# Loading and splitting the first layer's weights in another order at the start of a fused attention and MLP kernel

## What is computed

```
x = attention(q, k, v, mem_k, mem_v)   # 4 batches x 8 heads x 768 rows, head_dim 64; chunks of 32 rows,
                                       # each against 8 memory + 16 left + 32 own + 8 right keys, softmax
x = x as 3072 tokens x 512
h = x @ w_in                           # 512 x 2048
g = h * cos(h)
y = g @ w_out                          # 2048 x 512
m = max(y @ w1, y @ w2, y @ w3)        # 512 x 768 each
out = m @ w2_out                       # 768 x 512
```

## Time and profile before

| What | us |
|---|---|
| median of three runs | 960.74 |
| lowest and highest run | 957.79, 961.76 |
| the profiled execution, its own time | 957.79 |
| its span | 956.0 |
| PE busy in it | 937.4 (98%) |
| DVE busy | 678.0 (71%) |
| ACT busy | 512.6 (54%) |

### The profile page before, as it was taken

One profiled execution on the slowest core, in us unless ns is written; L12 is line 12 of the kernel. 1 busy time (PEld: TensorE's weight loads), 2 busy tenths in 40 slices (PEclk: granted clock), 3 DMA queues, 4 the chain that ended last, 5 costly groups with the idle time before them and its releaser, 6 DMA issues.

```text
span 956.0 us, 21412 instructions
## 1 busy us (share of the span) xinstructions
PE 937.4 (98%) x9100; PEld 918.7 (96%) x9100; DVE 678.0 (71%) x938; ACT 512.6 (54%) x689; POOL 183.2 (19%) x207
## 2 busy tenths in 40 slices
PE   6999999999999999999999999999999999999998
PEld 5889999999999999999999999999999999999997
DVE  5767666667666789989989889767446357677761
ACT  3879696978878894334343345433224224444541
POOL 0011211111111212001000003922000002683520
PEclk8999999999999999999999999999999999999999
DMA  8953446454653443444354343331120201335432
GB/s 302 367 190 130 154 163 212 149 189 160 203 179 124 137 168 123 154 132 156 119 196 150 113 138 97 116 122 65 60 97 34 99 34 56 129 115 171 171 111 88
DMA packets 55422, 135.60 MB, mean 142 GB/s; under 512 B 5152, under 2 KB 14368, under 8 KB 55328
## 3 DMA queue, kind: packets, MB, share of 16 engines
q1 hardware_dynamic: 44960, 98.58, 30.6%
q0 software_dynamic: 10368, 35.66, 10.3%
HBM read 87.03 MB, written 47.19 MB: 140 GB/s over the span
## 4 chain that ended last, share of the span: by engine, by line
PE 78%; ACT 8%; DVE 5%; DMA 5%; issue 2%; POOL 0%; SPq 0%; DVEq 0%; ACTq 0%
PE ps L604 25%; PE ps L606 24%; PE ps L605 24%; DMA g_dram<-work 3%; ACT work L871 2%; PE ps L645 1%; ACT work L876 1%; DVE units L1185 1%; ACT work L868 1%; PE ps L618 1%; PE ps L656 1%; ACT work L878 1%; DVE work L1148 1%; DMA early_qk<-qk_in 1%; PE ps L631 1%
## 5 line engine op out<-in xcount | busy, mean ns | idle before, releaser
L604 PE MATMUL ps<-units 128*128 128x384 f32 (+1 forms) x1940 | 607.0, 313 | 5.8 <-DVE units L1137 1.4
L606 PE MATMUL ps<-units 128*128 128x384 f32 (+1 forms) x1940 | 601.3, 310 | 0.0
L605 PE MATMUL ps<-units 128*128 128x384 f32 (+1 forms) x1940 | 601.1, 310 | 0.0
L604 PEld LDWEIGHTS ps<-units 128*128 128x128 f32 x1940 | 368.0, 190 | 10.6 <-DVE units L1089 1.7
L605 PEld LDWEIGHTS ps<-units 128*128 128x128 f32 x1940 | 368.2, 190 | 0.0
L606 PEld LDWEIGHTS ps<-units 128*128 128x128 f32 x1940 | 368.0, 190 | 0.0
L896 ACT CAST units<-work 128x1024 fp32r<-128x1024 f32 x96 | 85.8, 939 | 118.9 <-DVE work L1171 105.7
L1040 ACT COPY work<-ps 128x384 f32<-128x384 f32 (+1 forms) x144 | 63.5, 454 | 146.9 <-PE ps L606 146.7
L1185 DVE TENSOR_TENSOR units<-work,units 128x1024 fp32r<-128x1024 f32 x96 | 102.1, 1105 | 10.7 <-ACT units L896 10.7
L501 POOL DMA_DIRECT2D g_dram<-work x64 | 46.7, 729 | 300.9 <-DVE work L1148 295.2
L1148 DVE SCALAR_TENSOR_TENSOR work<-work 128x768 f32<-128x768 f32 x64 | 61.3, 958 | 39.1 <-ACT work L878 39.1
(11 more groups left out here) (91 smaller groups left out, 764.8 us busy)
## 6 DMA issues: line engine op xcount, KB each, us to landing
g_dram<-work POOLq DMA_DIRECT2D x64, 384.0 KB, 3.3
work<-g_dram SPq DMA_DIRECT2D x48, 512.0 KB, 3.7
work<-qk_in SPq DMA_DIRECT2D x18, 768.0 KB, 5.8
work<-w_in POOLq DMA_DIRECT2D x40, 256.0 KB, 4.0
h_dram<-work SPq DMA_DIRECT2D x24, 384.0 KB, 2.8
work<-h_dram SPq DMA_DIRECT2D x18, 512.0 KB, 3.8
work<-y_dram SPq DMA_DIRECT2D x8, 768.0 KB, 6.2
out<-work SPq DMA_DIRECT2D x24, 256.0 KB, 2.4
```

The source lines that it names most:

```text
L604: pe.matmul(o, wh, mh, start=start, stop=False, skip_group_check=onto)
L605: pe.matmul(o, wh, ml, start=False, stop=False, skip_group_check=onto)
L606: return pe.matmul(o, wl, mh, start=False, stop=stop, skip_group_check=onto)
```

## The change

It touches only orders; no operation is added or removed. In four places:

- **SP's queue.** The column groups 2 and 3 and the loads of pieces 3, 4 and 5 move up, the wait for the first weighted values (`pv_done`) ahead of them is gone, and the remaining groups are spread among them two by two. Each `load_qk` keeps its own wait for the scores of the piece whose buffer it takes.
- **The tables.** On ACT, column groups 6 to 15 are rounded at earlier steps, with the last at f = 4 in place of f = 9. On DVE, groups 5 to 15 move up in the same way, with the last at f = 8 in place of 10.
- **Ahead of the loop.** ACT rounds groups 2 and 3 between `x_high(0)` and `x_high(1)`. DVE does `x_low(0)` ahead of `normalise(2)` and `low_wi(1)` right behind it.
- **`normalise(n + 2)`** moves from step f = 11 to step f = 12, ahead of `x_low(n + 1)`, in blocks 0 to 6.

```
-HIGH_WI = (0, 0, 0, 0, 0, 0, 1, 1, 1, 5, 5, 5, 6, 7, 8, 9)
-LOW_WI = (0, 0, 0, 0, 0, 1, 2, 2, 3, 6, 6, 6, 7, 8, 9, 10)
+HIGH_WI = (0, 0, 0, 0, 0, 0, 0, 0, 1, 1, 2, 3, 3, 4, 4, 4)
+LOW_WI = (0, 0, 0, 0, 0, 0, 1, 1, 2, 3, 3, 4, 5, 6, 6, 8)
...
             load_v(1)
             load_v(2)
-            load_wi(0)
-            load_wi(1)
-            sp.wait_ge(pv_done, 1)
-            load_qk(NSUB)
-            load_qk(NSUB + 1)
-            for f in range(2, 6):
+            for f in range(4):
                 load_wi(f)
-            load_qk(NSUB + 2)
-            for f in range(6, 12):
-                load_wi(f)
+            for n in range(NSUB, 2 * NSUB):
+                load_qk(n)
+                load_wi(2 * n - 2)
+                load_wi(2 * n - 1)
+            load_wi(10)
+            load_wi(11)
             load_v(NSUB)
...
             x_high(0)
+            high_wi(2)
+            high_wi(3)
             x_high(1)
             x_high(2)
-            high_wi(2)
-            high_wi(3)
...
             low_wi(0)
+            x_low(0)
             normalise(2)
-            x_low(0)
+            low_wi(1)
             x_low(1)
             x_low(2)
-            low_wi(1)
             low_wi(2)
...
-                        if f == 11 and not last:
-                            normalise(n + 2)
-                        elif f == 13 and not last:
+                        if f == 13 and not last:
                             x_low(n + 2)
...
                         elif f == 12:
+                            normalise(n + 2)
                             x_low(n + 1)
```

## The result

The changed kernel is slower: 969.46 us in the median of 7 runs (963.63 to 970.4), against 960.89 of 7 runs of the kernel before (957.79 to 963.39). The ratio is 1.0075, with a 95% interval of 1.0055 to 1.0093, which is +7.2 us (5.3 to 8.9); the two medians by themselves lie 8.6 us apart. The forecast was 962.9, or +2.15, and its range ended at 967.2. A time over 965.5 had been given a chance of 0.13.

What follows compares the result with a forecast made beforehand. PE was taken to bound the kernel, with only its idle times in the first 62 us mattering. The terms +2.2 + 0.35 - 0.4 + 0 = +2.15 us on the median 960.74 gave 962.9 us, range 958.0 to 967.2.

Steps and rivals of the forecast that it cites:

- What bounds the kernel: Whole kernel: PE, busy 98% of the span; the change acts only through PE's idle time in the first 62 us.
- SP's queue, +2.2: Ahead of the loop: full DMA engines delay PE's instruction packet, new idle time near 17 us, +2.2 us, bounds 0 and 4.
- DVE ahead of the loop, +0.35: Ahead of the loop: x_low(0) first delays normalise(2) and all behind it, +0.35 us, bounds 0 and 0.6.
- The tables, -0.4: Block 0's loop: earlier rounding removes two idle times, later exponentials bring others; -0.4 us, bounds -2.06 and +0.8.
- the four priced terms: Block 0's loop: -2.06 us of idle times removed; +1.0 at turn_probs(3), +0.8 at f = 8, +0.4 at piece 4's values.
- normalise one step later, 0: Seven blocks: frees DVE for gated(4), needed only by a turn_out 2.1 us later; 0 us, bounds 0 and 7 x 0.1.
- No stop for instructions: Ahead of the loop: instructions reach PE in time, only -0.4 + 0.35 stay, 960.7 us; chance 0.25.
- All idle time of the loop won: Block 0's loop: ACT's five casts are hidden, the loop gives -2.06, no instruction stop, 959.0 us; chance 0.10.
- Stop and slow clock: Loop's start: a second idle time at 17.2 us brings PE's half clock into the first steps, 967.2 us; chance 0.15.

Runs made afterwards that it cites:

- e5: The changed kernel with WARM = 4 in place of 8, so fewer warm-up matmuls at PE's start: 968.94 us in one run.
- e3: The kernel before with SP's queue alone changed as in the change: 966.01 us, ratio 1.0031 to before.
- e4: The changed kernel with SP's wait for the first weighted values put back, behind the fourth column group: 966.75 us, ratio 1.0040 to before.
- e7: The kernel before with only DVE's order ahead of the loop as in the change: 960.26 us in one run.
- e12: The kernel before, unchanged, run for a third profile: 961.90 us.
- e2: The changed kernel with normalise(n + 2) put back to step 11: 966.56 us, ratio 1.0040 to before.
- e9: The changed kernel with normalise(n + 2) back at step 11 and SP's wait for the first weighted values back: 963.87 us, ratio 1.0013 to before.
- e6: The kernel before with only the two tables of the change: 963.93 us, ratio 1.0005 to before.
- e1: The kernel before with only normalise(n + 2) moved to step 12, ahead of x_low(n + 1): 966.88 us, ratio 1.0041 to before.
- e11: The kernel before with normalise(n + 2) moved to step 12 in blocks t = 2 and t = 4 only: 967.16 us in one run.
- e13: The kernel before, unchanged, run for a fourth profile: 965.81 us.
- e14: The changed kernel, unchanged, run for a second profile: 970.68 us.
- e15: The changed kernel, unchanged, run for a third profile: 969.39 us.
- e0: The kernel before, unchanged, run for a second profile: 962.74 us.
- e10: The kernel before with column groups 9 and 10 rounded earlier and one more wait on SP's queue ahead of load_v(1): 963.64 us, ratio 1.0006 to before.

## Why the prediction was wrong

- **What bounds the kernel: right in one half.** It is PE, and only idle times of PE count. But the forecast also had everything happen in the first 62 us, with PE running on by itself behind them. It had read this from one stretch, 60 to 80 us. The first pair of profiles grows apart by 2.7 us more in blocks 1 to 5.
- **SP's queue, +2.2 (bounds 0 and 4): right in mechanism and nearly in size.** The stop came, at the count that was worked out, with 1.94, 2.62 and 1.83 us in three profiles. e5 showed that it goes by the count of instructions, e3 and e4 that the loads make it. Timed alone the edit costs 3.0 us (0.9 to 5.0). What is over may be the clock, which stood at half in the loop's first 3 us in the changed kernel's first profile. By the profile that is 21.03 us of work from the loop's start to `turn_probs` (45.28 - 24.25) instead of 19.53 (41.58 - 22.05), 1.5 us, in that one execution. The forecast put a packet among full queues about 4 us behind one alone; its own numbers give 2 to 4 (3.2 to 4.7 against about 1), and no run here tells engines that take turns from any other way of sharing them.
- **DVE ahead of the loop, +0.35: right.** 0.62 instead of 0.2 us at the place named, and 0.41 us on the loop's start (e7 beside e12). Together with the queue +2.55 was forecast for the loop's start, and +2.4 measured on the average of the profiles.
- **The tables, -0.4 (bounds -2.06 and +0.8): the waits right, the sum not quite.** The waits that go and those that come are the ones named, 0.81, 0.48 and 0.41 for 1.0, 0.8 and 0.4. But the four priced terms add up to +0.14 as they stand, and -0.4 came from steps taken too short (2.1 us, where f = 8 took 2.33 before: 46.08 - 1.38 - 42.37). Alone the tables cost 0.5 us (-1.3 to +2.3). From the loop's start to the last `turn_out` of block 0 it is 39.9 us in e2, 40.3 in e9 and 41.9 in e6, against 39.8 in the first profile of before. The stop at the values of piece 4 was missed; it shows in six of the eight profiles with the new tables (0.58 to 1.21 us), and not in the changed kernel's first.
- **normalise one step later, 0 (bounds 0 and 0.7): this is the step that failed.** It measures +3.9 us alone (2.5 to 5.5), and 3.4 come back when it is undone. I had asked who needs `normalise`, and found a step of 2.1 us between. The question was what DVE does in the meantime: at its old place the operation filled a wait for ACT's square and cost little or nothing, at its new place it stands in full, 0.6 us, ahead of `x_low(n + 1)`, which the `turn_out` behind f = 13 needs. That it frees DVE for `gated` was true, and worth 0.2 us in block 1 and nothing in block 3, so `x_low` came 0.39 and 0.62 us later. The profile of before had the rows that showed it, `x_low` ending at 103.31 and PE's `turn_out` at 103.46, in block 1, which I took to have slack because PE was never idle there; my bound of 0.1 a block had no row behind it. The waits for `x_low` grow by 2.65 us on average (4.35 less 1.7). The other 1 us of the measured 3.4 to 3.9 isn't located; the wait of 1.97 us near 880, which came more often with this edit, would fill it, but that it belongs to the edit isn't shown.
- **Sum.** 3.9 + 3.0 + 0.5 = 7.4 us for the three edits timed alone, against 7.2 for the change. That they agree so closely is luck, since each of the three is known to 1.5 or 2 us. The gain is not hidden somewhere: the change adds its losses, and its one gain, the idle times in the loop, is paid back by ACT within block 0.
- **The rivals.** No stop for instructions: refuted by the stop of 1.94 us and by e5. All idle time of the loop won: refuted by the rows at 46.09 to 53.27. Stop and slow clock: happened in part, in two of the three profiles of the changed kernel, for about 3 us of the loop. It isn't bound to a second stop: e1, e11 and e13 have half clock from about 22.3 to 25.7 us without one, and e14 has the longest second stop, 2.62 us, and full clock in the loop. It is not what brought the time to 969; the range's upper end stood on it and was too low, since the term that failed had nearly no width.

## What to carry to other kernels

When an operation moves past a waiting one on the same engine, look at what the wait was hiding: an operation that fills a wait is free or nearly so, and the same one behind the wait costs most or all of its time to whatever comes next (0.39 and 0.62 us for an operation of 0.6 here), even if its own consumer is far away. An engine that is never idle can still be without slack, so compare the end of the last input with the start of its reader in every block through which an edit repeats. And earlier loads are not free where the instruction packets go through the same DMA engines, as the instruction queue's row in the page shows: before a pause in the loads is removed, see what came through in it.

## What the runs showed of the hardware

- **PE stopped in the middle of its small matmuls** at fixed counts of its records, 443, 696 and 1704, wherever in the work these fell; that it lacked instructions there is the reading that fits them. Counted from when PE's records reached a multiple of a packet, the next packet was read after about 1 us in the first profile of before at 14 us, where the DMA engines were quiet, and after 3 to 5 where they were full. Quiet engines don't make it sure: in e6 it took 2.5 to 3.5 us with the engines at 0.17 and less. PE went on 1.5 to 4 us after the reading (read at 17 to 18 and on at 19.45 in e15, 48 to 49 and 51.75 in e6).
- **GpSimd's subtraction of 128x256** took 0.74 us or 2.40 us for the same shape, in neighbouring instructions.
- **The start's clock** was different from one execution of the same kernel to the next: half from 11.6 to 18.5 us in the first profile of before, from 14.6 to 21.4 in e0 and from 10.1 to 16.9 in e12; in e7 and e9 it was full all the time from 10 to 30 us. The first stop was 1.4 to 2.3 us long over all profiles but e10's, and the profiles of the kernel before spread over 956.0 to 964.0 us of span. A single profile of either kernel could not have told their difference.
